# A chained MoE kernel: the search of the second routing in three steps a digit, four token tiles in one product

## The chip, the cores and the metric

One core of a Trainium2 chip runs the whole program. The metric is the device time of one execution in microseconds (us), and the median of several executions is compared.

## The reference

Three stages follow each other. Stage 1 is linear attention over 8 x 8 heads of 576 tokens, normed per head; stages 2 and 3 are mixtures of 8 experts (512 to 1024 to 512, relu) over the 4608 tokens. Stage 2 gives each token to its best expert. Stage 3 is greedy with a capacity, and its assignment is what the changed code computes:

```python
cap = N // E                                   # 576 rows per expert
order = np.argsort(-(x @ w_gate).flatten())
for idx in order:
    tok, e = (int(idx) // E, int(idx) % E)
    if assigned[tok] >= 0 or counts[e] >= cap:
        continue
    assigned[tok] = e
    counts[e] += 1
for e in range(E):
    mask = assigned == e
    out[mask] = np.maximum(x[mask] @ w1[e], 0.0) @ w2[e]
```

## The kernel before

**Stage 2.** The 4608 rows are sorted by expert into T1 = 43 tiles of 128. For each, TensorE does both layers in three passes of float32r parts (`in_parts`, L676: high x high, low weights x high, high weights x low), ScalarE (ACT) makes the high parts, relu and the copies, VectorE (DVE) the low parts and, by eight multiply-and-sum instructions a tile (`scores`, L1198), the second router's scores.

**The search.** The greedy assignment is done in 8 rounds (`select`, L1263, on DVE). In a round every open token bids for its best open expert (`bid`, one-hot, 43 tiles of 128 tokens), and a score is searched at which the first expert is full: 32 bits, four at a time, so R = 8 digits. A digit has two products on TensorE (`search`, L767). Step 1, count: for each of NTH = 15 thresholds, how many bids an expert has at or above it, less its room. That is 1 + 43 matmuls (L773, L775) with `bid` (its 8 columns in 128) as weights and `cmp` (15 columns) moving. DVE turns the counts into `ind` (L1301). Step 2, threshold: ones x `ind` (L778), after which DVE finds the digit (L1302 to L1313) and compares again (L1299). Three more steps end the round: the sums (L781, L782), the positions (L784, `mtot_h`), and the list of the 576 rows (43 matmuls, L787). So STEPS = 19. DVE asks through the semaphore `s_sel` (`ask`), TensorE answers through `s_selp`. After the sums the expert of the round is known (`expert_i`, L1336), and SP loads its weights (`load_phase`, L459: 8 pieces of 512 KB, at most two in flight). After the list POOL gathers its rows (L578).

**The phases.** Stage 3 is a phase per round, of T2 = 5 tiles. While TensorE does the phase of round kk, the search of round kk+1 runs beside it. The order is written by hand: a phase has 40 points, one behind every six 512-column matmuls (`in_parts` calls `point`); `gaps` says how many points lie between the steps of a search, and EARLY how many steps of it stand in the phase before the last. `searches` (L792) issues a step at its point, and TensorE waits there if DVE has not asked yet. The first tile of phase 0 has no second layer of a tile before it, so its points 4 to 7 follow each other with nothing between (L821). On DVE the low parts that a phase needs are "duties": `DUTIES` puts xT_lo and hT_lo, `LOW_BESIDE` the eight w_lo pieces, beside steps of the search (`beside_step`, L1250), after the ask and before the wait. Round 0 stands alone ahead of phase 0, and with it the first EARLY = 8 steps of round 1. DVE's rounds 2 to 7 are a loop of three times two.

Of the kernel before, what the change touches and what calls it, by code (L numbers as in the profile page):

```python
# [59 lines left out]
def build(nc, q, k, v, g_norm, w_gate, w_og, w1, w2, w_gate2, w21, w22, out, debug=None):  # L60
# [45 lines left out]

    LOW_BESIDE = [EARLY - 4, EARLY - 3, EARLY - 2, EARLY - 1, EARLY + 4, EARLY + 5, EARLY + 6, EARLY + 7]
    PIECES = len(LOW_BESIDE)

    with ExitStack() as ctx:  # L110
# [24 lines left out]
        ones_h = sb("ones_h", [P, P], F16)  # L135
        before = sb("before", [P, P])
# [4 lines left out]
        segment = sb("segment", [PT, E, G1])  # L141
# [16 lines left out]
        onehot = sb("onehot", [PT, E, G1])  # L158
# [57 lines left out]
        s_clear = sem("bids_cleared")  # L216
# [17 lines left out]
        s_sc = sem("scores_done")  # L234
        s_sel = sem("select_dve")
# [97 lines left out]
        bid = sb("bid", [P, T1, P], F16)  # L333
# [68 lines left out]
        def _(sp):  # L402
# [56 lines left out]
            def load_phase(kk, u):  # L459
# [27 lines left out]
        def _(pool):  # L487
# [84 lines left out]
            pool.memset(bid[:, :, :], 0.0).then_inc(s_clear, 1)  # L572
# [29 lines left out]
        def _(pe):  # L602
# [65 lines left out]
            for g in range(G1):  # L668
                if g % (G1 // 3) == 0:
                    pe.wait_ge(s_ohb, g // (G1 // 3) + 1)  # L670
                mm = pe.matmul(bank[2][:, 0:2 * T1], ohb[0:PT, g, :] if g < T1 else bid[0:PT, g - T1, :],
                               ra1[:, g, :, :], start=(g == 0), stop=(g == G1 - 1))
# [91 lines left out]

            cps, aps = sel_ps

            def search(kk, n):  # L767
# [3 lines left out]
                if n < 2 * R and n % 2 == 0:  # L771

                    pe.matmul(cps[:, 0:NTH], room_n[:, :], ones_h[:, 0:NTH], start=True, stop=False)  # L773
# [657 lines left out]
```

## Time and profile before

| | |
|---|---|
| median of 3 executions | 1497.14 us (1497.01 to 1498.32) |
| the profiled execution | 1500.03 us, span 1498.2 us |
| TensorE matmuls busy | 1315.6 us (88%) |
| VectorE busy | 974.1 us (65%) |
| ScalarE, GpSimd busy | 441.3 us, 397.5 us |
| granted TensorE clock, mean | 0.938 of full |

Stage 2 ends at about 793 us, phase 0 begins at 877 us, and the last phase ends at about 1482 us. The shares are means over stages that differ: between 794 and 877 us TensorE is nearly idle, in the phases it is nearly full. Matmuls are pipelined, so what a step costs is read from the distance of starts, not from durations.

### The profile page before, as it was taken

What the parts mean: (1) busy time and instruction counts of PE and PEld (TensorE: products, weight loads), DVE (VectorE), ACT (ScalarE), POOL (GpSimd) and SP (SyncE); (2) the same over time, 40 slices, a digit from 0 to 9 for tenths busy, and PEclk for the clock granted to TensorE, in tenths of its full rate; (3) what the DMA queues carried; (4) which work ended last, traced back from release to release, by engine and by line L of the source; (5) the groups of instructions that cost most, each with busy time, mean ns of one, the idle gap of its engine ahead of it and who ended that gap; (6) DMA issues with size and microseconds to landing.
All of it is one profiled execution on the core that took longest, in us unless ns stands there. A gap on an engine that the chain in (4) does not pass through costs nothing.

```text
span 1498.2 us, 26945 instructions
## 1 busy us (share of the span) xinstructions
PE 1315.6 (88%) x9724; PEld 1084.6 (72%) x9724; DVE 974.1 (65%) x2214; ACT 441.3 (29%) x784; POOL 397.5 (27%) x324
## 2 busy tenths in 40 slices
PE   5988718898999999999993169999999999999997
PEld 5877616786888888888882157878777777787885
DVE  1566793677567677776667768585758585767420
ACT  1655522122222222222220032423232323233431
POOL 1244426747616172480000001111111111111110
PEclk9989858999999999999996569999999999999999
DMA  9999128694514143241100304040404132222310
GB/s 218 253 271 289 57 45 297 220 352 154 156 43 155 42 157 106 89 146 49 43 22 15 124 18 148 30 152 30 145 30 132 50 117 65 82 93 84 104 32 18
DMA packets 71168, 173.48 MB, mean 116 GB/s; under 512 B 11624, under 2 KB 30136, under 8 KB 70400
## 3 DMA queue, kind: packets, MB, share of 16 engines
q1 hardware_dynamic: 46576, 108.61, 24.8%
q0 software_dynamic: 12368, 40.92, 8.6%
q10 hardware_dynamic: 12096, 22.19, 4.7%
q8 instruction: 87, 1.43, 0.4%
q14 instruction: 41, 0.34, 0.1%
HBM read 130.47 MB, written 41.23 MB: 115 GB/s over the span
## 4 chain that ended last, share of the span: by engine, by line
PE 67%; DVE 16%; DMA 6%; issue 5%; POOL 5%; ACT 1%; SPq 0%; DVEq 0%; POOLq 0%; ACTq 0%
PE bank L687 50%; PE bank L775 5%; PE bank L730 4%; POOL w_lo L524 3%; PE o_ps L648 2%; DMA xst<-x_rows,tok_i 2%; DMA x_sorted<-xst 1%; DMA v_sb<-in_v 1%; PE kv_ps L614 1%; POOL w_hi L522 1%; DMA w_sb<-in_moe_w 1%; PE bank L723 1%; PE bank L716 1%; DVE xrow L1052 1%; PE qt_ps L636 1%
## 5 line engine op out<-in xcount | busy, mean ns | idle before, releaser
L1202 DVE SCALAR_TENSOR_TENSOR bank<-bank,factor,wg2b 128x512 f32<-128x512 f32 x344 | 260.6, 758 | 10.8
L1189 DVE TENSOR_TENSOR hT_lo<-bank,hT_hi 128x512 fp32r<-128x512 f32 x166 | 107.0, 685 | 194.0 <-ACT hT_hi L932 185.0
L899 ACT ACTIVATE h<-bank 128x512 f32<-128x512 f32 x166 | 99.2, 598 | 356.8 <-PE bank L687 335.7
L687 PE MATMUL bank<-w_hi,xT_hi 128*128 (+1 forms) x664 | 193.1, 413 | 10.7 <-POOL w_lo L524 6.4
L687 PE MATMUL bank<-w_lo,xT_hi 128*128 (+1 forms) x664 | 190.6, 403 | 0.4 <-DVE w_lo L1237 0.4
L687 PE MATMUL bank<-w_hi,hT_hi 128*128 (+1 forms) x664 | 180.8, 411 | 6.2 <-DVE score L1205 3.3
L687 PE MATMUL bank<-w_hi,xT_lo 128*128 (+1 forms) x664 | 182.9, 397 | 0.0
L578 POOL DMA_INDIRECT xg<-y_rows,gat_i x40 | 41.6, 1040 | 502.3 <-DVE sca_i L1376 283.1
L687 PE MATMUL bank<-w_lo,hT_hi 128*128 (+1 forms) x664 | 173.4, 402 | 0.0
L687 PE MATMUL bank<-w_hi,hT_lo 128*128 (+1 forms) x664 | 171.0, 398 | 0.0
L687 PEld LDWEIGHTS bank<-w_hi,xT_lo 128*128 128x128 f32 x664 | 125.6, 189 | 30.5 <-issue 0.2
L687 PEld LDWEIGHTS bank<-w_lo,hT_hi 128*128 128x128 f32 x664 | 125.9, 191 | 29.4
L687 PEld LDWEIGHTS bank<-w_hi,hT_lo 128*128 128x128 f32 x664 | 124.2, 189 | 29.1
L687 PEld LDWEIGHTS bank<-w_hi,xT_hi 128*128 128x128 f32 x664 | 120.1, 193 | 33.8 <-issue 12.4
L687 PEld LDWEIGHTS bank<-w_lo,xT_hi 128*128 128x128 f32 x664 | 123.9, 191 | 28.0 <-DVE w_lo L1237 0.9
L687 PEld LDWEIGHTS bank<-w_hi,hT_hi 128*128 128x128 f32 x664 | 119.1, 191 | 28.2 <-issue 6.2
L524 POOL TENSOR_TENSOR w_lo<-w_sb,w_hi 128x1024 fp32r<-128x1024 f32 x56 | 134.3, 2398 | 4.5
L522 POOL CAST w_hi<-w_sb 128x1024 fp32r<-128x1024 f32 x56 | 58.3, 1041 | 183.0 <-DMA w_sb<-in_moe_w 183.0
L585 POOL DMA_INDIRECT out<-y,sca_i x40 | 44.8, 1120 | 230.2 <-ACT y L927 228.1
L1183 DVE TENSOR_TENSOR xT_lo<-bank,xT_hi 128x512 fp32r<-128x512 f32 x83 | 57.2, 690 | 72.6 <-ACT xT_hi L917 71.3
L932 ACT ACTIVATE hT_hi<-bank 128x512 fp32r<-128x512 f32 x166 | 90.8, 598 | 45.6 <-PE bank L730 33.7
L906 ACT ACTIVATE y<-bank,factor 128x512 f32<-128x512 f32 x43 | 29.5, 687 | 218.4 <-PE bank L687 193.5
(238 smaller groups left out, 1803.1 us busy)
## 6 DMA issues: line engine op xcount, KB each, us to landing
w_sb<-in_moe_w SPq DMA_DIRECT2D x112, 512.0 KB, 5.0
y_rows<-y ACTq DMA_DIRECT2D x43, 256.0 KB
x_sorted<-xst SPq DMA_DIRECT2D x41, 260.0 KB
xg<-x_sorted ACTq DMA_DIRECT2D x41, 260.0 KB
k_sb<-in_k SPq DMA_DIRECT2D x16, 576.0 KB, 15.5
v_sb<-in_v SPq DMA_DIRECT2D x16, 576.0 KB, 17.3
q_sb<-in_q SPq DMA_DIRECT2D x8, 1152.0 KB, 20.6
x_rows<-xrow POOLq DMA_DIRECT2D x16, 576.0 KB, 6.3
```

What stands on the lines that cost most here:

```text
L522: pool.tensor_copy(w_hi[:, 1 - e % 2, cols(i)], w_sb[:, e % 2, cols(i)]).then_inc(s_phi, 1)
L524: pool.tensor_tensor(w_lo[:, e % 2, cols(i)], w_sb[:, e % 2, cols(i)], w_hi[:, 1 - e % 2, cols(i)].bitcast(F32), ALU.subtract).then_inc(s_ ...
L578: pool.indirect_dma_start(out=xgs[w % 2][:, 0:DM], out_offset=None, in_=y_rows[:, :], in_offset=bass.IndirectOffsetOnAxis(ap=gat_i[:, w:w ...
L585: pool.indirect_dma_start(out=out[:, :], out_offset=bass.IndirectOffsetOnAxis(ap=sca_i[0:rows, w:w + 1], axis=0), in_=ys[w % 2][0:rows, :] ...
L687: mm = pe.matmul(ps, a[:, i % chunks, :], b[:, i % chunks, cols], start=(i == 0), stop=(i == 3 * chunks - 1))
L730: mm = pe.transpose(th_ps[half][:, i * P:(i + 1) * P], h[:, half * 4 + i:F:FC], ident[:, :])
L775: mm = pe.matmul(cps[:, 0:NTH], bid[:, g, :], cmp[:, g, :], start=False, stop=(g == T1 - 1))
L899: act.activation(h[:, half * HALF:(half + 1) * HALF], h_ps[half][:, :], ACT.Relu).then_inc(s_h, 1)
L932: act.activation(hT_hi[:, half * 4:(half + 1) * 4, :].rearrange("p a b -> p (a b)"), th_ps[half][:, :], ACT.Copy).then_inc(s_hT, 1)
L1183: dve.tensor_tensor(xT_lo[:, :, :].rearrange("p a b -> p (a b)"), tx_ps[:, :], xT_hi[:, :, :].rearrange("p a b -> p (a b)").bitcast(F32), ...
L1189: dve.tensor_tensor(hT_lo[:, half * 4:(half + 1) * 4, :].rearrange("p a b -> p (a b)"), th_ps[half][:, :], hT_hi[:, half * 4:(half + 1) * ...
L1202: ch.link(dve.scalar_tensor_tensor(out=prod_ps[:, :], in0=y1_ps[t % 2][:, :], scalar=factor[:, t:t + 1], in1=wg2b[:, e, :], op0=ALU.mult, ...
```

## The change

- A digit has three steps (STEPS = 27). The count multiplies four tiles at once: weights `bid` of 32 columns (4 tiles x 8 experts), moving `cmp` of 60 (4 tiles x 15), 11 matmuls. The result has the wanted counts in its diagonal blocks; DVE copies it (`dense`), and a second product of 1 + 4 small matmuls sums the blocks and takes off the room. Then the threshold product as before.
- `gaps` is one point between all steps up to the sums, EARLY is 3. So a phase holds steps 3 to 26 of the next round at points 0 to 21, 25 and 32, and steps 0 to 2 of the one after at points 37 to 39.
- Round 1 is wholly in phase 0, from point 2 on (`FIRST`), its last two steps at points 31 and 35; only round 0 stands ahead.
- Four w_lo pieces (round 0) or two (others) are made right behind the list (`behind_list`), the others beside steps.
- The last tile's scores come over TensorE: transposes of y, a copy, 4 matmuls with `wg2_sb`. The bids and the first compare of the first 40 tiles are made during the last tiles of stage 2, those of 3 tiles after.
- SP queues the 8 weight pieces of a phase without waiting between them.
- `bid` is 8 columns wide and no longer cleared by POOL.

```diff
-    STEPS = 2 * R + 3
-    EARLY = 8
-    gaps = [0] + [1, 2] * R + [4, 7]
+    STEPS = 3 * R + 3
+    EARLY = 3
+    GROUP = 4
+    gaps = [0] + [1, 1, 1] * R + [4, 7]
...
-    LOW_BESIDE = [EARLY - 4, EARLY - 3, EARLY - 2, EARLY - 1, EARLY + 4, EARLY + 5, EARLY + 6, EARLY + 7]
+    FIRST = [2 + n for n in range(3 * R)] + [27, 31, 35]
...
+    LOW_BEHIND_LIST = (0, 1)
+    LOW_BESIDE = {0: 2, 1: 3, 4: 4, 5: 5, 7: 6, 8: 7}
+    FIRST_LOW_BEHIND_LIST = (0, 1, 2, 3)
+    FIRST_LOW_BESIDE = {1: 4, 2: 5, 4: 6, 5: 7}
...
                 for i in range(PIECES):
                     w, at = (w21, i) if i < PIECES // 2 else (w22, i - PIECES // 2)
-                    wait_pos(sp, s_wp[i % 2], (kk * (PIECES // 2) + i // 2) * 16)
-                    alone(sp)
...
+            pe.wait_ge(s_y, T1)
+            for c in range(KC):
+                mm = pe.transpose(tx_ps[:, c * P:(c + 1) * P], ys[(T1 - 1) % 2][:, c * P:(c + 1) * P], ident[:, :])
+            mm.then_inc(s_yt, 1)
+            pe.wait_ge(s_ytc, 1)
+            for c in range(KC):
+                mm = pe.matmul(th_ps[0][:, 0:E], h[:, c * P:(c + 1) * P], wg2_sb[:, c, :], start=(c == 0), stop=(c == KC - 1))
...
-                    pe.matmul(cps[:, 0:NTH], room_n[:, :], ones_h[:, 0:NTH], start=True, stop=False)
-                    for g in range(T1):
-                        mm = pe.matmul(cps[:, 0:NTH], bid[:, g, :], cmp[:, g, :], start=False, stop=(g == T1 - 1))
...
+                if n < 3 * R and n % 3 == 0:
+                    for g in range(0, T1, GROUP):
+                        some = min(GROUP, T1 - g)
+                        mm = pe.matmul(dps[0:some * E, 0:some * NTH], bid[:, g:g + some, :].rearrange("p g e -> p (g e)"),
+                                       cmp[:, g:g + some, :].rearrange("p g n -> p (g n)"), start=(g == 0), stop=(g + GROUP >= T1))
+                elif n < 3 * R and n % 3 == 1:
+                    pe.matmul(cps[0:E, 0:NTH], room_n[:, :], ones_h[0:1, 0:NTH], start=True, stop=False)
+                    for g in range(GROUP):
+                        mm = pe.matmul(cps[0:E, 0:NTH], ident_h[:, g * E:(g + 1) * E], dense[:, g * NTH:(g + 1) * NTH],
+                                       start=False, stop=(g == GROUP - 1))
+                elif n < 3 * R:
+                    mm = pe.matmul(aps[:, 0:NTH], ones_h[0:E, :], ind[:, :], start=True, stop=True)
...
-            for n in range(EARLY):
-                search(1, n)
...
-                    ask(dve.tensor_scalar(ind[:, :], cps[:, 0:NTH], 0.0, None, ALU.is_ge))
+                    ask(compare(rest if first and r == 0 else every, thr))
+                    ask(dve.tensor_copy(dense[:, :], dps[0:GROUP * E, :]))
+                    ask(dve.tensor_scalar(ind[:, :], cps[0:E, 0:NTH], 0.0, None, ALU.is_ge))
...
+                behind_list(kk, u)
```

How the order changes, at three places. On TensorE, around the end of a search in phase 0, before the change (L687 are the tiles' matmuls, L723 and L730 transposes, L778 the last threshold product, L781 and L782 the sums):

```order
L778 MATMUL bank<-ind,ones_h 128x15
L687 MATMUL bank<-w_lo,xT_hi 128x512 x2
L687 MATMUL bank<-w_hi,xT_lo 128x512 x4
L723 MATMUL bank<-ident,xg 128x128 x4
L687 MATMUL bank<-w_hi,hT_hi 128x512 x6
L781 MATMUL bank<-sums_h,ones_h 128x16
L782 MATMUL bank<-sums_h,before_h 128x8
```

and the list of the same round with the first digit of the next, with the change (L708 are the tiles' matmuls, L744 and L751 transposes, L828 the list, L809 the count, L813 and L815 the second product, L819 the threshold product):

```order
L828 MATMUL bank<-ra,ohb 128x20 x43
L744 MATMUL bank<-ident,xg 128x128 x4
L708 MATMUL bank<-w_hi,hT_hi 128x512 x8
L708 MATMUL bank<-w_lo,hT_hi 128x512 x4
L809 MATMUL bank<-cmp,bid 32x60 x10
L809 MATMUL bank<-cmp,bid 24x45
L708 MATMUL bank<-w_lo,hT_hi 128x512 x4
L708 MATMUL bank<-w_hi,hT_lo 128x512 x2
L813 MATMUL bank<-ones_h,room_n 8x15
L815 MATMUL bank<-dense,ident_h 8x15 x4
L708 MATMUL bank<-w_hi,hT_lo 128x512 x6
L819 MATMUL bank<-ind,ones_h 128x15
```

Before, 12 matmuls and four transposes lay between a last threshold product and the sums. With the change every step is followed by six matmuls, and in phase 0 the transposes of the next phase's first rows (L744) come directly behind the list that names them.

On VectorE, from the copy of the list (L1371 before, L1451 now) to the next round's first compare, before and with the change:

```order
L1371 COPY lst<-bank 128x20
L1372 SCALAR_TENSOR_TENSOR gat_i<-lst 128x5
L1376 SCALAR_TENSOR_TENSOR sca_i<-lst 128x5
L1379 TENSOR_REDUCE m<-a 128x43
L1380 TENSOR_SCALAR m<-m 128x43
```

```order
L1451 COPY lst<-bank 128x20
L1452 SCALAR_TENSOR_TENSOR gat_i<-lst 128x5
L1456 SCALAR_TENSOR_TENSOR sca_i<-lst 128x5
L1307 TENSOR_TENSOR w_lo<-w_sb,w_hi 128x1024 x2
L1460 TENSOR_REDUCE m<-a 128x43
L1461 TENSOR_SCALAR m<-m 128x43
```

Two w_lo pieces now stand between the list and the score update (L1460 on), which ends in both versions with the branch back of the loop.

## Rows read from the trace of the kernel before

**Rows 1.** Windows: busy us of PE, PEld, DVE, ACT, POOL, then PEclk, DMA

```profile
793.50:877.20 83.70, 21.11 (x590) 18.36 (x590) 60.04 (x172) 7.01 (x8) 2.69 (x3) 0.52 0.19 61
953.00:1030.00 77.00, 75.33 (x708) 60.70 (x706) 54.73 (x129) 24.25 (x38) 10.68 (x10) 1.00 0.28 88
1086.00:1096.00 10.00, 7.84 (x81) 5.77 (x80) 6.00 (x16) 0.13 (x1) 0.54 (x1) 0.83 0.11 28
```

**Rows 2.** Timeline, stage 2 to search: start us, us, engine, line, what [idle before]

```profile
793.44 0.69 ACT L906 ACTIVATE y<-bank,factor 128x512 f32<-128x512 f32 x1 [6.05 <-PE bank L687]
...
803.64 0.49 DVE L1286 TENSOR_REDUCE best<-score 128x43 f32<-128x344 f32 x1
...
807.58 0.20 PE L773 MATMUL bank<-ones_h,room_n 128*128 128x15 f16 x1 [14.18 <-DVE cmp L1299]
```

**Rows 3.** Timeline, a digit of round 0, TensorE

```profile
813.12 0.20 PE L778 MATMUL bank<-ind,ones_h 128*128 128x15 f16 x1 [0.27 <-DVE ind L1301]
...
815.00 0.20 PE L773 MATMUL bank<-ones_h,room_n 128*128 128x15 f16 x1 [1.68 <-DVE cmp L1299]
```

**Rows 4.** Timeline, from round 0's expert to phase 0

```profile
839.58 0.14 DVE L1336 TENSOR_SCALAR expert_i<-sc 1x1 int32<-1x1 f32 x1
...
856.06 0.17 DVE L1376 SCALAR_TENSOR_TENSOR sca_i<-lst 128x5 int32<-128x5 f32 x1
...
861.19 5.79 ACT L939 ACTIVATE w_hi<-w_sb 128x1024 fp32r<-128x1024 f32 x6 [67.06 <-SPq L473]
...
877.28 2.05 PE L687 MATMUL bank<-w_hi,xT_hi 128*128 128x512 f32 x4 [0.78 <-ACT xT_hi L917]
```

**Rows 5.** Timeline, TensorE's matmuls around two steps in phase 1

```profile
1016.08 1.14 PE L730 MATMUL bank<-ident,h 128*128 128x128 f32 x8
...
1017.99 0.63 PE L687 MATMUL bank<-w_lo,xT_hi 128*128 128x512 f32 x2
...
1019.04 1.09 PE L687 MATMUL bank<-w_hi,xT_lo 128*128 128x512 f32 x4
...
1020.91 0.63 PE L687 MATMUL bank<-w_lo,xT_hi 128*128 128x512 f32 x2
...
1023.05 1.09 PE L687 MATMUL bank<-w_hi,xT_lo 128*128 128x512 f32 x4
```

**Rows 6.** TensorE's waits from 877 to 1475: us in total, times, longest us

```profile
PE bank L773 <- DVE cmp L1299: 7.3, 3, 3.6
```

**Rows 7.** Timeline, TensorE, the end of a search in phase 2

```profile
1054.39 0.18 PE L778 MATMUL bank<-ind,ones_h 128*128 128x15 f16 x1
...
1058.45 0.18 PE L781 MATMUL bank<-sums_h,ones_h 128*128 128x16 f16 x1 [0.51 <-DVE sums_h L1324]
...
1066.25 0.18 PE L784 MATMUL bank<-mtot_h,before_h 128*128 128x1 f16 x1 [1.01 <-DVE mtot_h L1356]
```

**Rows 8.** List to gather (timeline), and the gather's landing (instructions of L578)

```profile
1001.16 0.18 DVE L1371 COPY lst<-bank 128x20 f32<-128x20 f32 x1 [1.44 <-PE bank L787]
...
1002.21 0.97 POOL L578 DMA_INDIRECT xg<-y_rows,gat_i  x1 [14.04 <-DVE sca_i L1376]
...
1006.92 0.83 DVE L1299 TENSOR_TENSOR cmp<-best,thr 128x645 f16<-128x645 f32 x1
...
DMA to landing us min/median/max: 3.3/3.4/5.1
```

**Rows 9.** The page's 40 slices, bytes moved

```profile
GB/s 218 253 271 289 57 45 297 220 352 154 156 43 155 42 157 106 89 146 49 43 22 15 124 18 148 30 152 30 145 30 132 50 117 65 82 93 84 104 32 18
```

**Rows 10.** ScalarE at a phase's start (timeline), and VectorE's groups by line, phase 2

```profile
1040.03 1.99 ACT L939 ACTIVATE w_hi<-w_sb 128x1024 fp32r<-128x1024 f32 x2
...
L1237 DVE TENSOR_TENSOR w_lo<-w_sb,w_hi 128x1024 fp32r<-128x1024 f32 x7 | 8.5, 1219 | 0.0
```

**Rows 11.** Timeline, VectorE's branch back in phase 2, and TensorE

```profile
1084.48 0.16 DVE L1285 TENSOR_SCALAR room_n<-room 1x8 f16<-1x8 f32 x1 [3.96 <-issue]
...
1088.51 0.18 PE L773 MATMUL bank<-ones_h,room_n 128*128 128x15 f16 x1 [2.15 <-DVE cmp L1299]
```

More of the change, by code:

```diff
@@ L104, in build @@
     assert all(n != EARLY or ("x", T2 - 1) not in d for n, d in DUTIES.items())
-    LOW_BESIDE = [EARLY - 4, EARLY - 3, EARLY - 2, EARLY - 1, EARLY + 4, EARLY + 5, EARLY + 6, EARLY + 7]
-    PIECES = len(LOW_BESIDE)
+    FIRST = [2 + n for n in range(3 * R)] + [27, 31, 35]
+    assert len(FIRST) == STEPS and FIRST[-1] < POINTS[-EARLY]
+    FIRST_DUTIES = {n: [] for n in range(STEPS)}
+    for g in range(T2):
+        for kind, due, need in (("h", 8 * g, 8 * g + 5), ("x", 8 * g + 4, 8 * g + 8)):
+            if (kind, g) != ("h", 0) and all((kind, g) not in DUTIES[n] for n in range(EARLY)):
+                p = min(x for x in FIRST if x >= due)
+                assert p <= need
+                FIRST_DUTIES[FIRST.index(p)].append((kind, g))
+    PIECES = 8
+    LOW_BEHIND_LIST = (0, 1)
+    LOW_BESIDE = {0: 2, 1: 3, 4: 4, 5: 5, 7: 6, 8: 7}
+    FIRST_LOW_BEHIND_LIST = (0, 1, 2, 3)
+    FIRST_LOW_BESIDE = {1: 4, 2: 5, 4: 6, 5: 7}
     with ExitStack() as ctx:
@@ L792, in searches @@
             def searches(kk, i):
+                first = isinstance(kk, int) and kk == 0
+                if first and i in FIRST:
+                    search(1, FIRST.index(i))
                 if i in POINTS:
@@ L797, in searches @@
                     ahead = kk + 1 if n < STEPS else kk + 2
-                    if not (isinstance(kk, int) and ahead >= E):
+                    if not (first and ahead == 1) and not (isinstance(kk, int) and ahead >= E):
                         search(ahead, n % STEPS)
@@ L1205, in scores, with bid_on, compare, less_room @@
                 dve.tensor_scalar(score[:, t, :], sc_raw[:, :], cap_v[:, t:t + 1], None, ALU.min).then_inc(s_sc, 1)
+            def bid_on(gs):
+                n = gs.stop - gs.start
+                full = [P, n, E]
+                link(dve.tensor_reduce(best[:, gs], score[:, gs, :], AX, ALU.max))
+                ch.inc(dve.tensor_scalar(m43[:, 1, gs], best[:, gs], -INPLAY, 100.0, ALU.is_lt, ALU.mult))
+                link(dve.tensor_tensor(a3[:, gs, :], score[:, gs, :], best[:, gs].unsqueeze(2).to_broadcast(full), ALU.is_equal))
+                link(dve.tensor_tensor(a3[:, gs, :], a3[:, gs, :], rank8[:, :].unsqueeze(1).to_broadcast(full), ALU.mult))
+                link(dve.tensor_reduce(m43[:, 0, gs], a3[:, gs, :], AX, ALU.max))
+                link(dve.tensor_tensor(m43[:, 0, gs], m43[:, 0, gs], m43[:, 1, gs], ALU.add))
+                link(dve.tensor_tensor(bid[:, gs, :], a3[:, gs, :], m43[:, 0, gs].unsqueeze(2).to_broadcast(full), ALU.is_equal))
+            def compare(gs, thr):
+                full = [P, gs.stop - gs.start, NTH]
+                return dve.tensor_tensor(cmp[:, gs, :], best[:, gs].unsqueeze(2).to_broadcast(full),
+                                         thr.bitcast(F32).unsqueeze(1).to_broadcast(full), ALU.is_ge)
+            def less_room():
+                ch.inc(dve.tensor_scalar(room_n[:, :], room[0:1, :], -1.0, None, ALU.mult))
+            known = slice(0, T1 - 3)
+            rest = slice(T1 - 3, T1)
             factor_kept(0)
@@ L1209, in _ @@
             first_low(range(PIECES // 2, PIECES))
-            for t in range(T1 + 2):
+            for t in range(T1 + 1):
                 if t > 2:
```

167 lines of the change are left out of this document (97 added, 70 removed).

## The prediction

> **What bounds the kernel now.** I read the busy shares by stage first. From the end of the first mixture's last tile to the first matmul of phase 0 TensorE has next to nothing to do: 83.7 us at a granted clock of 0.52, while VectorE is busy for 60.0 of them [rows 1]. In the phases it is the other way round: in 77.0 us TensorE is busy for 75.3 at full clock and VectorE for 54.7 [rows 1]. So the exposed stretch is bound by the chain VectorE-TensorE of search 0, and each phase by TensorE's matmuls, with VectorE as a partner that must answer in time.
>
> The rows of the exposed stretch give its parts: VectorE still scores two tiles after the last matmul (y of the last one is made at 793.44), and the first count product starts at 807.58 [rows 2]; from a digit's threshold product to the next digit's count it takes 1.88 us, of which VectorE has all but the two handovers [rows 3]; expert 0 is known at 839.58, the list is there at 856.06, the weights at 861.19, and the first matmul of phase 0 starts at 877.28 [rows 4]. The last 15 us hold eight steps of search 1.
>
> In the phases, I read what a step of the search costs TensorE. Eight L687 matmuls without a step take 1020.91 - 1019.04 = 1.87 us, four 0.93. Around a threshold product four take 1019.04 - 1017.99 = 1.05, so it costs 0.12; around a count product (1+43 matmuls) 1023.05 - 1020.91 = 2.14, so it costs 1.21 [rows 5]. A digit costs 1.33 us. The difference of the two steps, 1.09 us for 43 more matmuls, is 0.025 each, which leaves 0.09 per step as fixed. TensorE waits for the search little: the largest line from phase 0 to the end is 7.3 us in three waits [rows 6]; the waits for the sums and for mtot are 0.5 and 1.0 in each of seven phases [rows 7], and with some small ones it is 20 us.
>
> **The change, part by part.** Differences are against the profiled execution (1500.03 us, 1498.2 span); the median of the runs shown is 2.9 us lower, so I add the sum to 1497.1.
>
> *Start of search 0.* Tile 42's eight VectorE products go; its score comes over TensorE: y is there at 794.13 [rows 2], then 4 transposes, a copy on ACT, 4 matmuls and a minimum, about 3 us by the sizes of such rows here (0.6 each for copy and transposes), so 797.2. VectorE's own scores of tile 41 are done by then. Bids and compare, from 803.64 to the product 3.9 us [rows 2], are then made for three tiles, not 43: some 1.9 us. The first count starts at about 799.1: 8.5 us earlier. The work on the 40 known tiles (some 3.7 us) lies in VectorE's idle time in the first mixture's last tiles, where it waits for ACT: nothing, and some microseconds if that cover is short. A digit: 11 matmuls for 44 saves 1.0 us, the added copy and second product cost 0.2 + 0.35 and two handovers; I take 0.1 us less per digit. The list is there about 9.5 us earlier, at 846.6.
>
> *Start of phase 0.* The eight exposed steps of search 1 move beside phase 0. Next is late: the gather of y, which follows the list within a microsecond and lands 3.4 us (at most 5.1) after its issue [rows 8], so 850.6; then transposes, ACT's copy and the first matmul, some 1.8 us: **852.4, 24.9 us earlier** than 877.28. Weights: expert known at 830.1, and from there to the first w_hi it took 21.6 us with two pieces in flight [rows 4]. With all eight queued, 4.19 MB at the best slice (352 GB/s, [rows 9]) would be 12 us. At 13 and one for the issue, six w_hi are done by 850; if nothing is gained, phase 0 starts 5 us later.
>
> *Steps in the phases.* The new digit has 11 + 5 + 1 matmuls: 0.42 + 0.24 + 0.12 = 0.78 us at 0.03 each. No row shows a count product with 32 columns of weights and 60 moving ones. Below: 0.025, the rate of the 43 now. Above: the float transposes of L730, eight of 128 columns in 1.14 [rows 5] with their end, so some 0.12 each; 60 of 128 columns of that is 0.055. I take 0.03, near the f16 rows. Digits inside the phases: 4 + 6 x 8 = 52 now, 56 then. 52 x 1.33 = 69.2 against 56 x 0.78 = 43.7: **25.5 us less.** Bounds: 28 less, and 11 less (11 x 0.025 more in 56 digits).
> The Trainium skill (TensorE: Matmul & The Clock Gate, Back-to-back issue gap) gives a stream of weight-load and matmul pairs 81 ns a pair at 128 columns. As an estimate from that page, 16 pairs a digit would cost 0.8 us more, and the change lose some 45 us more. The 44 pairs of a count product here, though with 15 columns, cost 1.21 us [rows 5], which speaks against it.
>
> *Waits in the phases.* This term decides. Before, a digit had its count and its threshold product on two points of a grid of six matmuls (1.40 us), and two points in between for VectorE. Now every point has a step, and the sums' product comes one point after the last threshold product. I laid the instructions of one regular phase on a time line by rows; TensorE's waits:
> - From a threshold product to the next count it takes 815.00 - 813.12 = 1.88 us [rows 3]; TensorE is there after 1.40 + 0.14. Four such gaps at 0.3: 1.2. (Where transposes lie in the gap, none.)
> - Twice a duty in between is late. At the phase's start ACT does two w_hi (1.99) before xT_hi [rows 10]; xT_lo and w_lo sit before VectorE's next answers: 0.9. One tile later hT_lo waits for ACT: 1.1.
> - Sums: 1054.39 to 1058.45 is 4.06 [rows 7]; TensorE had 3.4 us of work and waited 0.51; now it has 1.5: 2.5. Totals to mtot: 7.8 less the xT_lo that is now elsewhere, 7.1 to 7.3 [rows 7], against 6.4 of work: 0.9.
> - The list comes nine points later. From the list's copy to the gather's issue is 1.05 us, to its landing 4.5 to 4.7; TensorE reaches those rows in some 4: 0.8 with the gather's spread. Two w_lo (1.22 each, [rows 10]) are put before the score update; list to first compare took 1007.75 - 1001.16 = 6.6 us [rows 8] and takes 8.9, TensorE needs 8.2: 0.7.
> Sum: 8 us a regular phase (1, 3, 5), before 1.5. Phases 2 and 4: at the branch back of its loop VectorE sat idle for 3.96 us ("issue"), of which TensorE now feels 2.15 [rows 11]. With no slack left it feels all: 12. Phase 6: 7. Phase 0: points 4 to 7 of its first tile have no matmuls in between, since no second layer precedes it (that was the 3.6 of [rows 6]); now four steps stand there, and the search begins late behind four w_lo: 1.0 + 2.1 + 7.5; then 1.2 for gaps, 1.0 sums, 1.2 mtot, 2.4 list; the gather directly behind the list 4.8; and 1.2: 22.
> Total 22 + 3 x 8 + 2 x 12 + 7 + 1 = 78 against 20: **58 us more.**
>
> *Clock.* After the wait in phase 2 of [rows 11] the same matmuls ran at half rate for some microseconds: 0.83 over the ten [rows 1], 1.7 us. It happened three times after the start. Now four waits are that long or longer (1.7 more), and each of seven waits before the sums, of 2.5 us, may do it; I take three of them, 5 us. **6 us more.**
>
> *Weights queued at once.* In a regular phase they come 12 to 20 us after the expert. Up to 16 nothing waits; at 20 ACT's w_hi block the relu, some 2 to 4 us a phase.
>
> Sum: -24.9 - 25.5 + 58 + 6 = +13.6 us: **1511.**
>
> **Rivals.**
> A. *Every wait before the sums drops the clock.* For: 2.5 us is more than the 2.15 that did it. Against: a wait of 1.0 never did (clock 1.00 in regular phases, [rows 1]). Seven times 1.7 in place of 5: +7, 1518.
> [...]
> B. *VectorE keeps up, faster than before.* If the waits at single digits and behind duties vanish because TensorE's other delays let VectorE get ahead, what is left is 2.5 + 0.9 + 1.5 a phase, and half of phase 0's: 78 becomes about 48, and the clock term 2. That gives -21, 1476 at best, about 1487 with half of it. It decides from the point where all waits together are below 65 us. For: each wait delays TensorE and not VectorE. Against: the chain is serial; VectorE can't start its answer before the product that it answers.
> C. *The new count product is slow*, 0.055 a matmul: +15, 1526.
> D. *Queued pieces come no sooner than now*, so that weights are late in each phase: +5 and 7 x 2 to 4, about 1535.
> E. *The waits are right but the start gains less*, or cancels them: within 3 us of 1497.
>
> **Chances.** Forecast 0.50 (1503 to 1517), A 0.15, B 0.17, C 0.07, D 0.06, E 0.05. A measurement here can tell about 0.2%, 3 us. Faster 0.17, same 0.05, slower 0.78. The range leaves out D, most of B and the far half of C: 1494 to 1523.
>
> **What would show it.** Right: first matmul of phase 0 at about 852; regular phases some 79 to 81 us long in place of 76.8; waits of TensorE for sums_h of 2.4 us each, seven times; a wait for a DMA of 4 to 5 us in phase 0; count groups of about 0.35 us. Wrong: regular phases under 77 us, a wait for sums_h under 1 us, or a first matmul after 858. The weakest part is the 78 us of waits; an error of a quarter there changes the sign.

## The result, and the profile after

| | before | after |
|---|---|---|
| median | 1497.73 us (1497.01 to 1502.44, 4 runs) | 1535.41 us (1533.09 to 1536.54, 4 runs) |
| span of the profiled execution | 1498.2 us | 1534.5 us |

The ratio is 1.0239, with an interval of 1.0212 to 1.0266: slower by 36 us. Forecast were 14 us, in a range that ended at 1523.

The exposed stretch, the time between stage 2 and phase 0, in the timeline after (start us, us, engine, line, what, idle before and what ended it):

```profile
804.55 0.72 PE L809 MATMUL bank<-cmp,bid 128*32 128x60 f16 x11 [2.11 <-DVE cmp L1263]
...
807.96 0.72 PE L809 MATMUL bank<-cmp,bid 128*32 128x60 f16 x11 [1.67 <-DVE cmp L1263]
...
832.12 0.14 DVE L1413 TENSOR_SCALAR expert_i<-sc 1x1 int32<-1x1 f32 x1
846.87 5.79 ACT L981 ACTIVATE w_hi<-w_sb 128x1024 fp32r<-128x1024 f32 x6 [49.19 <-SPq L494]
848.41 0.17 DVE L1456 SCALAR_TENSOR_TENSOR sca_i<-lst 128x5 int32<-128x5 f32 x1
852.97 1.13 PE L744 MATMUL bank<-ident,xg 128*128 128x128 f32 x4 [5.01 <-DMA xg<-y_rows,gat_i]
854.87 2.05 PE L708 MATMUL bank<-w_hi,xT_hi 128*128 128x512 f32 x4 [0.78 <-ACT xT_hi L959]
```

A digit of round 0 takes 807.96 - 804.55 = 3.41 us; between the same products it took 3.48 before. Phase 0 starts at 854.87, where it started at 877.28 [rows 4]: 22.4 us earlier, 24.9 were forecast. From the expert to the first w_hi it is 846.87 - 832.12 = 14.75 us, not 21.6, so the queued pieces do come sooner, and the last thing that phase 0 waits for is the gather.

Everything behind that is worse. Windows from one round's list product to the next one's, first without, then with a branch back of VectorE's loop in it (columns: PE, PEld, DVE, ACT, POOL busy, PEclk, DMA share, GB/s):

```profile
1016.10:1098.70 82.60, 76.99 (x483) 57.04 (x482) 55.97 (x137) 24.32 (x39) 10.74 (x10) 0.98 0.24 82
1098.70:1186.50 87.80, 78.47 (x483) 58.08 (x482) 56.18 (x137) 24.48 (x39) 10.79 (x10) 0.96 0.23 77
```

The first takes 82.6 us (79 to 81 were forecast); the same stretch of the kernel before took 76.7 (999.9 to 1076.6, clock 1.00). TensorE's waits from 855 us to the end (in total, times, longest):

```profile
PE bank L809 <- DVE cmp L1263: 22.5, 29, 5.9
PE bank L822 <- DVE sums_h L1401: 14.1, 7, 2.3
PE bank L744 <- DMA xg<-y_rows,gat_i: 10.3, 7, 4.3
PE bank L819 <- DVE ind L1378: 4.3, 7, 0.9
PE bank L708 <- ACT w_hi L981: 2.4, 1, 2.4
PE bank L828 <- DVE ra L1449: 2.3, 1, 2.3
```

With the small ones they are 58.9 us, against 20.2 before (where [rows 6] was the largest line). The gather, never waited for before, now costs TensorE 10.3 us. The branch back of VectorE's loop:

```profile
1108.66 0.16 DVE L1267 TENSOR_SCALAR room_n<-room 1x8 f16<-1x8 f32 x1 [3.70 <-issue]
...
1112.77 0.47 PE L809 MATMUL bank<-cmp,bid 128*32 128x60 f16 x11 [3.97 <-DVE cmp L1263]
```

TensorE waited 2.15 us there in [rows 11], now it waits for all of the idle time and more (3.97 against 3.70). And the clock, behind a wait for the sums in phase 0:

```profile
996.66 0.18 PE L822 MATMUL bank<-sums_h,ones_h 128*128 128x16 f16 x1 [2.15 <-DVE sums_h L1401]
...
998.18 3.15 PE L708 MATMUL bank<-w_hi,hT_lo 128*128 128x512 f32 x8
1001.16 1.05 PE L751 MATMUL bank<-ident,h 128*128 128x128 f32 x8
```

Eight matmuls take 3.15 us where eight at 2.4 GHz take 2.03: a part of them ran at the 1.2 GHz level. Over all such groups behind the start of phase 0, what they take beyond 0.234 us a matmul is, as an estimate, 18.5 us; before it was 6.1. The granted clock itself says how long TensorE was at the 1.2 GHz level in the phases: 50.2 us in all, 18.7 before.

Last the steps. TensorE's timeline in phase 1 around a threshold, a count and a second product:

```profile
1029.69 0.63 PE L708 MATMUL bank<-w_hi,hT_lo 128*128 128x512 f32 x2
1030.25 0.18 PE L819 MATMUL bank<-ind,ones_h 8*128 8x15 f16 x1
1030.36 1.15 PE L751 MATMUL bank<-ident,h 128*128 128x128 f32 x8
...
1032.28 0.62 PE L708 MATMUL bank<-w_lo,xT_hi 128*128 128x512 f32 x2
1032.89 0.47 PE L809 MATMUL bank<-cmp,bid 128*32 128x60 f16 x11
1033.29 0.73 PE L708 MATMUL bank<-w_lo,xT_hi 128*128 128x512 f32 x2
1033.86 1.10 PE L708 MATMUL bank<-w_hi,xT_lo 128*128 128x512 f32 x4
1034.88 0.17 PE L813 MATMUL bank<-ones_h,room_n 1*8 1x15 f16 x1
1034.91 0.24 PE L815 MATMUL bank<-dense,ident_h 32*8 32x15 f16 x4
1035.08 1.20 PE L708 MATMUL bank<-w_hi,xT_hi 128*128 128x512 f32 x4
```

From 1029.69 to 1030.36 are 0.67 us, with two matmuls (0.47): the threshold costs 0.20. From 1033.86 to 1035.08 are 1.22, with four matmuls (0.93): the second product costs 0.29. From 1032.28 to 1033.86 are 1.58, with four matmuls on both sides of the count, so it costs 0.65 there. I took the difference up to the first row behind the step at every step behind 950 us at which the timeline shows no wait (it leaves out idle time under 0.15 us). Medians, for steps between two groups of L708:

| step | before | after |
|---|---|---|
| count | 1.13 (44 matmuls) | 0.57 (11 matmuls) |
| second product | | 0.29 (5 matmuls) |
| threshold | 0.04 | 0.20 |

The same threshold product, one matmul of 15 columns, costs 0.16 us more. What differs is its form: before it was ones (128 rows) x `ind`, now `8*128`, eight rows of the array. Two things are not in this table. In front of a count TensorE is often idle for up to 0.15 us; where it has no idle time at all, the count costs 0.50. And behind every step the first L708 matmul is followed after 0.32 us and not after 0.23: 0.08 more, and 0.11 more behind a product on a part of the array. The forecast's prices [rows 5] hold this delay. In its measure a digit is 1.13 + 0.04 + 2 x 0.08 = 1.33 us before, just as it said, and 0.50 + 0.29 + 0.20 + 3 x 0.105 = 1.31 after, where it said 0.78. (The expectations below use 1.37 for the changed kernel, from a few rows with some idle time.) From row to row, and with the steps beside transposes, which are dearer in both kernels, the mean digit is 1.22 us before and 1.17 after.

### The profile page after: what moved, and what is told of

Read it like the earlier page. It is cut to its first block, busy times and chain, and to the rows that moved or that the text cites. A ratio compares the mean times of both kernels' runs of the same rounds, so it can differ in the third digit from the quotient of the medians.

```text
span 1534.5 us, 23543 instructions
## 1 busy us (share of the span) xinstructions
PE 1326.5 (86%) x7944; PEld 1055.6 (69%) x7944; DVE 981.7 (64%) x2268; ACT 444.5 (29%) x785; POOL 393.2 (26%) x323
## 4 chain that ended last, share of the span: by engine, by line
PE 61%; DVE 15%; DMA 7%; issue 7%; POOL 6%; ACT 2%; SPq 1%; DVEq 0%; POOLq 0%; ACTq 0%
PE bank L708 47%; PE bank L751 4%; POOL w_lo L545 2%; DVE cmp L1263 2%; DMA xst<-x_rows,tok_i 2%; PE bank L809 2%; DMA w_sb<-in_moe_w 2%; PE o_ps L669 2%; DVE w_lo L1307 1%; DMA x_sorted<-xst 1%; DMA v_sb<-in_v 1%; POOL xrow L553 1%; POOL w_hi L543 1%; PE bank L744 1%; ACT w_hi L981 1%
## 5 line engine op out<-in xcount | busy, mean ns | idle before, releaser
L1245 DVE SCALAR_TENSOR_TENSOR bank<-bank,factor,wg2b 128x512 f32<-128x512 f32 x336 | 254.6, 758 | 10.4
L708 PE MATMUL bank<-w_hi,xT_hi 128*128 (+1 forms) x664 | 195.1, 416 | 13.7 <-POOL w_lo L545 8.3
L708 PE MATMUL bank<-w_lo,xT_hi 128*128 (+1 forms) x664 | 197.8, 408 | 0.0
L599 POOL DMA_INDIRECT xg<-y_rows,gat_i x40 | 47.3, 1182 | 571.3 <-DVE sca_i L1456 429.7
L708 PE MATMUL bank<-w_hi,hT_hi 128*128 (+1 forms) x664 | 183.5, 414 | 6.9 <-DVE score L1248 4.7
L708 PE MATMUL bank<-w_hi,xT_lo 128*128 (+1 forms) x664 | 183.0, 397 | 0.0
L708 PE MATMUL bank<-w_hi,hT_lo 128*128 (+1 forms) x664 | 181.2, 412 | 0.0
L708 PE MATMUL bank<-w_lo,hT_hi 128*128 (+1 forms) x664 | 178.6, 405 | 0.0
L708 PEld LDWEIGHTS bank<-w_hi,hT_lo 128*128 128x128 f32 x664 | 129.2, 197 | 31.0
L708 PEld LDWEIGHTS bank<-w_hi,xT_lo 128*128 128x128 f32 x664 | 125.8, 189 | 30.5
L708 PEld LDWEIGHTS bank<-w_lo,hT_hi 128*128 128x128 f32 x664 | 124.5, 191 | 29.0
L708 PEld LDWEIGHTS bank<-w_hi,xT_hi 128*128 128x128 f32 x664 | 119.3, 193 | 36.4 <-issue 15.3
L708 PEld LDWEIGHTS bank<-w_lo,xT_hi 128*128 128x128 f32 x664 | 123.2, 191 | 27.8
L708 PEld LDWEIGHTS bank<-w_hi,hT_hi 128*128 128x128 f32 x664 | 120.3, 193 | 29.5 <-issue 6.5
L969 ACT ACTIVATE y<-bank 128x512 f32<-128x512 f32 x40 | 23.9, 598 | 260.9 <-PE bank L708 260.9
```

The lines of the kernel that those rows point to most:

```text
L599: pool.indirect_dma_start(out=xgs[w % 2][:, 0:DM], out_offset=None, in_=y_rows[:, :], in_offset=bass.IndirectOffsetOnAxis(ap=gat_i[:, w:w ...
L708: mm = pe.matmul(ps, a[:, i % chunks, :], b[:, i % chunks, cols], start=(i == 0), stop=(i == 3 * chunks - 1))
L1245: ch.link(dve.scalar_tensor_tensor(out=prod_ps[:, :], in0=y1_ps[t % 2][:, :], scalar=factor[:, t:t + 1], in1=wg2b[:, e, :], op0=ALU.mult, ...
```

## The experiments

Three theories were set up for what a digit costs too much. **S**: a product on a part of the array costs about 0.2 us more where it meets products on the whole of it. **H**: every further handover costs that, whatever its form. **M**: the 60 moving columns set the price. Each ratio is to the kernel before, run on the same chip, where its median was 1502.84 us beside runs 1 to 4, 1500.25 beside 5 to 8, 1499.26 beside 9 and 10, and 1500.08 beside 11. So medians of different groups can differ by some us through the chip; the ratios are free of that. Spans are of one profiled execution each.

**1. Threshold on the whole array.**

```diff
-                    mm = pe.matmul(aps[:, 0:NTH], ones_h[0:E, :], ind[:, :], start=True, stop=True)
+                    mm = pe.matmul(aps[:, 0:NTH], ones_h[:, :], ind[:, :], start=True, stop=True)
```
(`ind` has 128 rows again, the others zero.)

> The changed kernel with its threshold product on the whole array (128 rows of ones and ind, rows 8 to 127 of ind zero), as in the kernel before. Theory S (a product that uses part of the array costs about 0.2 us more where it meets the tiles' full matmuls: 0.09 before it and 0.10 behind it): the step falls from 0.31 to 0.12 us, and over 56 digits in the phases the time falls by 10 to 11 us, to about 1525. Rival H (each further handover costs, whatever its shape): no change, 1535.

Measured: 1529.47 us, ratio 1.0181 (1.0155 to 1.0206), span 1526.0, 8.5 less than after; 10 to 11 were expected. In the traces, the steps and the delays behind them take 9.7 us less, the time at the lower clock costs 5.5 less, and the waits grow by 6.8.

**2. Count on the whole array.** The weights of the count are 128 columns of `bid` (16 tiles) in place of 32; the rows of the result that are not wanted are not read.

```diff
-mm = pe.matmul(dps[0:some * E, 0:some * NTH], bid[:, g:g + some, :].rearrange("p g e -> p (g e)"),
+mm = pe.matmul(dps[:, 0:some * NTH], bid[:, g:g + P // E, :].rearrange("p g e -> p (g e)"),
```

> The changed kernel with the count product's weights 128 columns wide (32 wanted, the others are the next tiles' bids, and their rows of the result are not read). Theory S: the step falls from 0.65 to about 0.42 us, the time by 11 to 13 us, to about 1523. Rival M (the 60 moving columns set the price of a matmul here): at most 1 us less. Rival H: no change.

Measured: 1529.62 us, ratio 1.0186 (1.0164 to 1.0207), span 1523.3, 11.2 less; by the ratios it is 8 less, where 11 to 13 were expected.

**3. All three on the whole array**: both edits, and the second product with zeros around `room_n`, `dense` and `ident_h`.

```diff
-mm = pe.matmul(cps[0:E, 0:NTH], ident_h[:, g * E:(g + 1) * E], dense[:, g * NTH:(g + 1) * NTH],
+mm = pe.matmul(cps[:, 0:NTH], ident_h[:, g * E:g * E + P], dense[:, g * NTH:(g + 1) * NTH],
```

> All three products of a digit on the whole array (the second one with 128 x 128 weights too, its other rows zero or not read). Theory S: 33 us less, about 1502, the step costs 0.42 + 0.24 + 0.12 us a digit as the prediction had them. The waits grow back by a few us, since TensorE reaches the steps earlier. Rival H: no change, 1535.

Measured: 1515.85 us, ratio 1.0099 (1.0071 to 1.0127), span 1513.4, 21.1 less than after. Expected were 33 less, so this is a miss in size. The second product at the place shown above for the changed kernel:

```profile
1024.73 1.09 PE L708 MATMUL bank<-w_hi,xT_lo 128*128 128x512 f32 x4
1025.66 0.18 PE L813 MATMUL bank<-ones_h,room_n 128*128 128x15 f16 x1
1025.70 0.25 PE L815 MATMUL bank<-dense,ident_h 128*128 128x15 f16 x4
1025.80 1.18 PE L708 MATMUL bank<-w_hi,xT_hi 128*128 128x512 f32 x4
```

It costs 1.07 - 0.93 = 0.14 us here and 0.29 there.

**4. The other way round**, the kernel before with a threshold product of eight rows.

```diff
-mm = pe.matmul(aps[:, 0:NTH], ones_h[:, :], ind[:, :], start=True, stop=True)
+mm = pe.matmul(aps[:, 0:NTH], ones_h[0:E, :], ind[0:E, :], start=True, stop=True)
```

> The kernel before with its threshold product made narrow (8 rows of ones and of ind), nothing else. Theory S: the step goes from 0.12 to 0.31 us, 52 of them in the phases, so 8 to 10 us slower than before, about 1506. Rival H: no change, 1497.

Measured: 1509.75 us, ratio 1.0062 (1.0038 to 1.0086), span 1507.0. Nothing is added here, only the form changes, and it costs 8.8 us of span. Of these, 1.9 lie ahead of phase 0; in the phases the steps and the delays behind them take 8.9 us more (0.16 and 0.02 for each of the 52 thresholds is 9.4), and the clock gives 2 back. H alone can't do that. The weight loads (PEld) show where it goes; first of this kernel, then of the kernel before:

```profile
1015.00 0.89 PEld L687 LDWEIGHTS bank<-w_lo,hT_hi 128*128 128x128 f32 x4
1016.25 0.09 PEld L778 LDWEIGHTS bank<-ind,ones_h 8*128 8x128 f16 x1 [0.36 <-issue]
1016.36 0.76 PEld L687 LDWEIGHTS bank<-w_lo,hT_hi 128*128 128x128 f32 x4
```

```profile
1010.87 0.89 PEld L687 LDWEIGHTS bank<-w_lo,hT_hi 128*128 128x128 f32 x4
1012.03 0.10 PEld L778 LDWEIGHTS bank<-ind,ones_h 128*128 128x128 f16 x1 [0.27 <-issue]
1012.04 0.77 PEld L687 LDWEIGHTS bank<-w_lo,hT_hi 128*128 128x128 f32 x4
```

The load of the small product starts 0.09 later, and the next one follows it by 0.11 us in place of 0.01. The Trainium skill (TensorEngine Tiling (Array Packing), Key Properties) says that "Changing tiling mode (not just tile) drains the TensorE". The traces agree in one respect: the price is nearly the same for one product (0.16), five (0.15) and eleven (0.17), as a price of going over to the other form and back would be, and not one of each product. That a product on a part of the array counts as such a mode, and that a drain is what happens there, no run shows.

By form, medians as above:

| step | after | 1 | 2 | 3 |
|---|---|---|---|---|
| count | 0.57 | 0.57 | 0.40 | 0.41 |
| second | 0.29 | 0.29 | 0.29 | 0.14 |
| threshold | 0.20 | 0.04 | 0.20 | 0.04 |

Each part falls only where its form is changed, so S holds. M does not: the count of 11 products with the same 60 moving columns costs 0.41 on the whole array, and 0.33 where TensorE has no idle time in front of it (0.50 on a part), which is 0.030 each. And for H little is left: a whole-array step of one product costs 0.04 and the 0.08 behind it, the 0.12 that the forecast had. No run tried other sizes, so from how many rows or columns on a product is cheap is open.

Run 3 gained 21 us. From the two traces, the steps take 23.5 us less and the delays behind them 2.2, and phase 0 starts 2.3 earlier; TensorE's waits grew from 58.9 to 65.7: a faster TensorE meets the same chain of VectorE. The clock cost about the same. What remains is 15 us above the kernel before, so the waits came next.

**5. The sums one point later**, on the kernel of run 3.

```diff
-    gaps = [0] + [1, 1, 1] * R + [4, 7]
+    gaps = [0] + [1] * (3 * R - 1) + [2, 4, 6]
```

> The kernel with all three products over the whole array, and its sums step two places behind the last threshold instead of one (gaps 2, 4, 6 in place of 1, 4, 7; the list keeps its place). There TensorE waited for the sums 14.9 us in seven waits of up to 2.4 us, and after most of them ran its matmuls at half rate. Theory (the wait is VectorE's chain between the last threshold and the sums, one place too short): six or seven waits fall from 2.3 to about 0.5, which is -12 us, some 3 to 5 come back at the positions step, and with the clock staying up another 0 to -10: 1499 to 1508 against 1515.9 of its base. Rival (the whole chain from the last digit to the list is the bound, so the wait only moves): 1513 to 1517.

Measured: 1506.37 us, ratio 1.0046 (1.0025 to 1.0067), span 1501.7, 11.7 less than run 3. The waits of run 3 and of this run:

```profile
PE bank L809 <- DVE cmp L1267: 27.4, 41, 6.1
PE bank L822 <- DVE sums_h L1406: 14.9, 7, 2.4
...
PE bank L825 <- DVE mtot_h L1441: 1.1, 1, 1.1
```

```profile
PE bank L809 <- DVE cmp L1267: 27.2, 41, 6.1
...
PE bank L822 <- DVE sums_h L1406: 7.0, 7, 1.0
PE bank L825 <- DVE mtot_h L1441: 6.2, 7, 1.1
```

The waits for the sums halved, but 5.1 of the 7.9 us came back at the positions: the rival was right on that, and all waits fell by 3 us only (65.7 to 62.3). The time is in the theory's range all the same, since the gain came from the clock. No wait for the sums is longer than 1.0 now, what the matmuls take beyond full speed fell from 20.2 to 8.0 us, and the time at the 1.2 GHz level from 54.5 to 27.0. In run 3 the clock fell at each of the six waits of 2.3 to 2.4 us for the sums, here at none of them.

**6. The load waits put back**, on the changed kernel.

```diff
+                    wait_pos(sp, s_wp[i % 2], (kk * (PIECES // 2) + i // 2) * 16)
+                    alone(sp)
                     sp.dma_start(w_sb[:, u, i * w_piece:(i + 1) * w_piece],
```

> The changed kernel with the weight pieces issued as before, each waiting for the piece two ahead of it. If queueing them at once brought the weights sooner, each round's high pieces are 3 to 5 us later now, and TensorE, which waits 2.4 us for them once in the changed kernel, waits in most phases: 1545 to 1560. If the pieces came no sooner (rival D of the prediction): 1532 to 1538, with no new waits for w_hi.

Measured: 1566.89 us, ratio 1.0449 (1.0396 to 1.0502), span 1559.3. That is above the range of 1545 to 1560. The prediction's rival D is out: in this order the queued pieces are worth some 25 to 31 us. But the new waits are not where I expected them. TensorE waits for `cmp`, and VectorE for ACT's w_hi; its line after, and here:

```profile
DVE w_lo L1307 <- ACT w_hi L981: 1.0, 1, 1.0
```

```profile
DVE w_lo L1309 <- ACT w_hi L983: 23.0, 7, 5.6
```

The pieces that VectorE makes behind the list wait for late weights, and the score update and the next round's bids stand behind them. TensorE waits 42.4 us for `cmp`, where it was 22.5.

**7. Start and order without the three steps.** The changed start, FIRST, EARLY = 3 and the pieces behind the list, but two steps a digit, on the whole array.

```diff
-    STEPS = 3 * R + 3
-    gaps = [0] + [1, 1, 1] * R + [4, 7]
+    STEPS = 2 * R + 3
+    gaps = [0] + [1, 2] * R + [4, 7]
```

> The changed kernel's start and its order of rounds (round 1 wholly inside phase 0, three steps of a round ahead of its phase), but the digit in two steps as before: 44 products on the whole array, then the threshold, 19 handovers a round instead of 27, 1.33 us a digit against the 1.37 measured in the changed kernel. Theory L (the waits come from the order: the round ahead ends close before its phase, its list, the updates and the low pieces follow each other on VectorE): the waits of the phases stay near 5 in the even ones and 9 in the others, and the time is 1512 to 1522. Rival T (the waits come from the third handover of each digit): waits fall to those of before, about 1.5 and 3.5 a phase, and the time is 1488 to 1497, under the kernel before by the earlier start.

Measured: 1531.01 us, ratio 1.0194 (1.0148 to 1.024), span 1535.3. The waits behind the start of phase 0 are 53 us. From list to list they are 5.8, 8.7 (3.5 of it for w_hi) and 5.3 without a branch back, 9.0 and 8.9 with one, as theory L has it; the low clock costs 24 us (70.7 at the 1.2 GHz level), more than it had, which may be what puts the time above its range. Rival T is out: with this order and none of the new products the kernel is almost as slow as the changed one.

**8. Another order with the wide products.** Six steps of round 1 ahead of phase 0, the list at point 29, pieces beside the steps, none behind the list. The start of round 0 of the changed kernel stays, and so do the products on the whole array of run 3.

```diff
-    EARLY = 3
-    gaps = [0] + [1, 1, 1] * R + [4, 7]
-    LOW_BEHIND_LIST = (0, 1)
-    LOW_BESIDE = {0: 2, 1: 3, 4: 4, 5: 5, 7: 6, 8: 7}
+    EARLY = 6
+    gaps = [0, 1, 1] + [2] + [1] * (3 * R - 4) + [2, 4, 6]
+    LOW_BESIDE = {1: 0, 3: 1, 4: 2, 5: 3, 8: 4, 9: 5, 13: 6, 15: 7}
```

> Wide products in three steps (about 0.6 us a digit in the phases), but an order of rounds between the two kernels: six steps of round 1 ahead of phase 0, every round's list 29 places into its phase (the changed kernel has it at 32, the kernel before at 23), the sums two places behind the last digit, low pieces beside the steps and none behind the list. From the kernel before: the start -6 (the last tile's score over TensorE and the bids of the known tiles ahead), steps 54 digits by 0.75 less, -40, waits up from some 16 us to 35 with 27 handovers instead of 19, +19, clock +4: 1498 - 23 = 1475, between 1468 and 1485. Rival (three handovers a digit always cost what they do in the changed kernel, some 59 us of waits and a lower clock): 1498 to 1506.

Measured: 1483.16 us, ratio 0.9877 (0.9831 to 0.9924), span 1481.3: faster than both kernels, inside the 1468 to 1485 that were expected. Behind the start of phase 0:

```profile
PE bank L795 <- DVE cmp L1252: 16.1, 33, 4.0
PE bank L811 <- DVE mtot_h L1416: 8.4, 7, 1.3
PE bank L808 <- DVE sums_h L1381: 7.1, 7, 1.1
```

No line for the gather is left. All waits are 39 us, and the lower clock costs 7.

**9. The same order, products on parts of the array again** (the three edits of runs 1 to 3 undone; one of them:)

```diff
-mm = pe.matmul(aps[:, 0:NTH], ones_h[:, :], ind[:, :], start=True, stop=True)
+mm = pe.matmul(aps[:, 0:NTH], ones_h[0:E, :], ind[:, :], start=True, stop=True)
```

> The kernel of the run before this one called best, with the three products of a digit on parts of the array again, as the changed kernel has them (32 output columns for the count, 8 for the second, 8 rows for the threshold); its order of rounds stays. Theory S (each such product costs some 0.2 us more where it meets matmuls of the whole array): 54 digits in the phases by 0.4 to 0.8 us, +21 to +35, less 3 to 5 of waits that shrink: 1500 to 1515. Rival (the price only shows where VectorE is late and the weights can't be loaded ahead, as in the changed kernel's order): under 1492.

Measured: 1503.6 us, ratio 1.0032 (1.0007 to 1.0056), span 1499.9. The form of the products alone is worth 20 us here too (23 by the ratios, 18.6 by the spans), on an order in which VectorE is hardly late (waits 34 us). The rival is out.

**10. The start alone**: the kernel before, its order and its two steps, with the changed start of round 0 and the queued loads. Against run 7:

```diff
-    EARLY = 3
+    EARLY = 8
-    LOW_BEHIND_LIST = (0, 1)
-    LOW_BESIDE = {0: 2, 1: 3, 3: 4, 4: 5, 5: 6, 6: 7}
+    LOW_BESIDE = {4: 0, 5: 1, 6: 2, 7: 3, 12: 4, 13: 5, 14: 6, 15: 7}
```

> The kernel before with the changed start alone: the last tile's scores by TensorE, bids and first comparison of 40 tiles ahead, weight pieces issued without waits; two steps a digit, eight steps of a round ahead of its phase, gaps, low pieces as before, all products on the whole array. The search of round 0 starts 6.4 us sooner (the last score at 797.16 and 0.2 for each of eight short operations, against 803.64 for the first long one), nothing else is later: 1490 to 1495 against 1500 of the runs before. Rival (the weights of round 0 or the gather take it back): 1497 to 1501.

Measured: 1492.59 us, ratio 0.994 (0.9914 to 0.9965): 6.7 us faster than the 1499.26 of the kernel before, as expected. The ratio makes it 9, and the profiled executions 3.6, with phase 0 4.3 earlier.

**11. Pieces beside the steps**, on the kernel of run 5.

```diff
-    LOW_BEHIND_LIST = (0, 1)
-    LOW_BESIDE = {0: 2, 1: 3, 4: 4, 5: 5, 7: 6, 8: 7}
+    LOW_BEHIND_LIST = ()
+    LOW_BESIDE = {0: (0, 1), 1: (2,), 2: (3,), 4: (4,), 5: (5,), 7: (6,), 8: (7,)}
```

> The run wide_all_sums_later with the two low pieces that VectorE makes behind each later round's list put beside the next round's first steps instead (two beside the first, one each beside the second and third). If these pieces in front of the score update cause the changed order's waits, TensorE waits 2.4 us less for the first comparison of the rounds that follow the loop's branch back and 0.3 to 1 less elsewhere, some of it given back at the first digit's second step: -3 to -8, 1498 to 1503 against 1506.4. Rival (they only lie in time that VectorE has, and the next answers come later instead): 1504 to 1509.

Measured: 1500.24 us, ratio 1.0000 (0.9981 to 1.0019), against 1.0046 of run 5: about 6 us less (7 by the ratios, give or take 4), inside the expectation. From 855 us on TensorE's waits for `cmp` fell from 27.2 to 24.4 and those for the gather from 10.7 to 6.2; 2.7 came back at the second product, and all of them fell from 62 to 58. The pieces behind the list are a part of the order's cost, and not the largest.

The runs side by side, from each trace: span, start of phase 0, TensorE's waits behind it, what its matmuls there took beyond full speed (an estimate), and the time there at the 1.2 GHz level.

| kernel | span | phase 0 at | waits | low clock costs | at 1.2 GHz |
|---|---|---|---|---|---|
| before | 1498.2 | 877.3 | 20.2 | 6.1 | 18.7 |
| after | 1534.5 | 854.9 | 58.9 | 18.5 | 50.2 |
| 3, whole array | 1513.4 | 852.6 | 65.7 | 20.2 | 54.5 |
| 5, sums later | 1501.7 | 853.9 | 62.3 | 8.0 | 27.0 |
| 6, load waits | 1559.3 | 858.0 | 74.7 | 26.2 | 72.2 |
| 7, order, two steps | 1535.3 | 858.1 | 53.2 | 24.3 | 70.7 |
| 8, another order | 1481.3 | 863.8 | 39.0 | 7.2 | 18.1 |
| 9, that order, part of array | 1499.9 | 859.6 | 33.8 | 8.6 | 20.7 |

## Why the prediction was wrong in its size

The direction was right: the waits of the new order cost more than the earlier start gives. But the sum was 23 us short, because a saving that it counted on did not come. Term by term, in the difference of the two profiled executions (+36.3):

| term | forecast | measured |
|---|---|---|
| start of phase 0 | -24.9 | -22.4 |
| steps in the phases, from row to row | -25.5 for this and the next | +2 |
| the delay behind each step | | +7 |
| waits | +58 | +38.7 |
| clock | +6 | +11 |

*Steps in the phases* is the term that failed. It reads "The new digit has 11 + 5 + 1 matmuls: 0.42 + 0.24 + 0.12 = 0.78 us at 0.03 each". In that measure the digit is 1.31 us. The rate of 0.03 a matmul, where I put the doubt, was right for products on the whole array: 0.33 + 0.08 = 0.41 for the count, where the forecast had 0.42. The fixed cost of a step was taken as 0.09 whatever its form, and the bounds, 28 and 11 less (by their own sum 10), covered only the rate. All three products of the new digit stand on a part of the array, and each costs 0.15 to 0.2 us more for it (runs 1 to 4 and 9). Without it a digit is 0.33 + 0.14 + 0.04 + 3 x 0.08 = 0.75 us, so the forecast's 0.78 was the price of a kernel that wasn't this one. In the mean over run 3 the form is worth some 0.46 a digit, 56 digits, about 26 us. No row of the trace of before had such a product between whole ones, so the bound had to come from somewhere else than [rows 5]; I gave none. That leaves 9 of the 35 us by which the term was off. They go with waits: the prices were read where TensorE runs on, and a step that ends a wait costs more beyond the wait itself (a count of run 3 with 0.94 us of wait takes 1.43 in all, so 0.49 in place of 0.33; transposes 0.67 behind a wait for the gather, 0.39 without, six times). How much of the 9 that is was not added up.

*Waits* were forecast too high, 58 more for 38.7. That the total was 23 us off and not over 40 is luck: these 19 us too many stood against the 35 too few of the steps. From list to list they are 5.6, 9.0 and 4.9 without a branch back (8 were forecast; 2.4 of the 9.0 is for w_hi, which was not), 9.3 and 8.7 with one (forecast 12). The waits for mtot mostly did not appear. The sums had 2.5 in the forecast and 2.1 to 2.3 in six of seven rounds; the gather 0.8 and 0.9 to 1.1; the branch back was felt in full, as forecast. The errors of the two terms lean against each other: a dearer step gives VectorE time, and with whole-array products (run 3) the waits are 65.7.

*Clock* was 11 for 6 (12.4 by the rougher estimate of the table above). Rival A had the better of it: the clock fell at five of the six waits of 2.2 us for the sums, and run 5 shows that the clock more than the waiting was what they cost. It is no sure thing: runs 1 and 2 had six such waits each, and the clock fell at two. Waits of 2.15 to 2.4 us were followed by the lower clock in 15 of 24 cases (after and runs 1 to 3), and waits of 1.0 (run 5) in none. The Trainium skill (TensorE: Matmul & The Clock Gate, Why this matters for your kernels) warns of idle gaps between bursts of matmuls, but of longer ones than these. Here the shorter ones were often enough, and the measurement decides.

*Start and loads* were right within 3 us, and rival D was wrong: the pieces came in 14.75 us, the forecast had 14. Rival B was right in part on the waits: all of them together are 58.9 us, under its mark of 65, and 5.6 and 4.9 in two regular phases, where it had 4.9. Its time, 1476 to about 1487, was out all the same, since the steps saved nothing and the clock cost 11 us and not 2. Rival C's price of 0.055 a matmul seemed to come true for the count (0.57 / 11 = 0.052), but for another reason: the same 60 columns on the whole array cost 0.030. The Trainium skill (TensorE: Matmul & The Clock Gate, Back-to-back issue gap) has 81 ns a pair at 128 columns; the pairs of 15 and 60 columns here are far below it.

What did the parts of the change bring? In medians, with what the ratios make of it in brackets: the start by itself -6.7 us (-9) (run 10); the three steps on the whole array in a milder order another -9.4, from 1492.6 to 1483.2 (-9) (run 8); putting them on parts of the array +20.4 (+23) (run 9); and the changed order +31.8, from 1503.6 to 1535.4 (+31), though it starts phase 0 some 5 us earlier. That order is several things at once: round 1 wholly inside phase 0, each list three points later, the sums one point behind the last threshold (8 to 12 us less when moved, run 5), two pieces behind the list (6 us, run 11). How the rest divides was not tried.

## What to carry to other kernels

In this kernel a small matmul between large ones was priced by its form before its size. So try it on the whole array, with zeros or unread rows around it, where a few of them stand alone in a stream of whole-array matmuls. When a step's cost is worked out from rows, ask which property of the row (rows and columns of the array, engine state before and behind) the new step doesn't share, and let the bounds cover that. The order that started phase 0 sooner paid once and cost in every round that followed; count both before the step's own savings.

## What the runs showed of the hardware

- A step of products on 8 rows, on 32 columns, or on 32 rows and 8 columns of the array costs 0.15 to 0.2 us more between whole-array products than the same step on all of it (runs 1 to 4, 9), be it 1, 5 or 11 products; for the 8 rows of run 4, 0.09 of it before the weight load and 0.10 behind. A single whole-array f16 product of 15 columns costs 0.04.
- Behind every step the first large matmul is followed 0.08 us later than usual (0.32 for 0.23), 0.11 behind products on a part of the array. With 51 more steps this is 7 us.
- Eleven pairs of weight load (128 columns) and f16 product of 60 columns cost 0.33 us, 0.030 each; 44 pairs with 15 columns 1.13, so 0.026 each. Four times the columns cost 1.2 times as much a pair.
- Waits of 2.15 to 2.4 us in front of the sums brought the clock down to the 1.2 GHz level in five of six cases (after), six of six (run 3) and two of six each (runs 1 and 2); those of at most 1.0 in run 5 in none of seven. Between these it is open: in the kernel before the clock fell behind a wait of 1.57 us for the count, in run 4 it did not behind two of 1.6 and 1.7.
